# The fifth matmul of the first product on 64 array rows, two output tiles side by side

## What is computed

```python
w = exp(weight_gen - max);  w = w / (sum(w) + 1e-9)         # 8 heads, 7 taps
x = sum over 7 taps of w * (x shifted by the tap)            # 8192 x 192
h = maximum(x @ w_in1, 0);  x = (h * h) @ w_out1             # 192 -> 2048 -> 192
h = x @ w_in2;              out = (h * clip(h + 3, 0, 6) / 6) @ w_out2
```

## Time and profile before

| | |
|---|---|
| median of 3 runs | 1269.47 us |
| span of the profiled execution | 1266.2 us |
| TensorE matmul busy | 1228.9 us, 5536 matmuls |
| TensorE weight loads busy (beside the matmuls) | 1002.4 us |
| VectorE busy | 911.6 us |
| ScalarE busy | 655.9 us |
| GpSimd busy | 43.0 us |
| matmuls of the first product (line 601) | 2640 |

### The profile page before, as it was taken

One profiled execution on the slowest core, in us unless ns is written; L12 is line 12 of the kernel. 1 busy time (PEld: TensorE's weight loads), 2 busy tenths in 40 slices (PEclk: granted clock), 3 DMA queues, 4 the chain that ended last, 5 costly groups with the idle time before them and its releaser, 6 DMA issues.

```text
span 1266.2 us, 14912 instructions
## 1 busy us (share of the span) xinstructions
PE 1228.9 (97%) x5536; PEld 1002.4 (79%) x5536; DVE 911.6 (72%) x930; ACT 655.9 (52%) x732; POOL 43.0 (3%) x31
## 2 busy tenths in 40 slices
PE   2898999999999999999999999999999999999998
PEld 1886888888888888888888888888888888888886
DVE  8869777786777867677686777867677686776554
ACT  3774555545555554554555455454555545555554
POOL 4124000000000000000000000000000000000000
PEclk9899999999999999999999999999999999999999
DMA  5410000010000100000000000100000000000000
GB/s 154 128 44 17 32 17 32 0 45 2 16 31 0 47 0 16 31 16 31 0 27 20 16 31 0 47 0 16 31 16 31 0 16 31 12 0 1 13 1 25
DMA packets 12802, 31.43 MB, mean 25 GB/s; under 512 B 1140, under 2 KB 7666, under 8 KB 12784
## 3 DMA queue, kind: packets, MB, share of 16 engines
q1 hardware_dynamic: 12784, 31.19, 7.6%
HBM read 24.89 MB, written 6.29 MB: 25 GB/s over the span
## 4 chain that ended last, share of the span: by engine, by line
PE 92%; DVE 6%; issue 1%; ACT 1%; DMA 0%; SPq 0%; DVEq 0%; ACTq 0%
PE h_ps L601 45%; PE y_ps L622 9%; PE y_ps L627 9%; PE y_ps L624 9%; PE y_ps L623 9%; PE y_ps L626 9%; DVE acc L430 2%; DVE hid_lo L496 1%; DVE prod L443 1%; DVE hid L485 1%; PE y_ps L637 1%; PE y_ps L638 1%; PE y_ps L648 1%; PE y_ps L652 0%; DMA xwin<-in_x_dram 0%
## 5 line engine op out<-in xcount | busy, mean ns | idle before, releaser
L601 PE MATMUL h_ps<-xt,win 128*128 128x512 f32 (+1 forms) x2640 | 643.3, 390 | 1.4 <-DVE xt L478 1.4
L601 PEld LDWEIGHTS h_ps<-xt,win 128*128 128x128 f32 x2640 | 487.8, 190 | 109.2 <-DVE xt L478 1.8
L496 DVE TENSOR_TENSOR hid_lo<-hid,hid_hi 128x1024 fp32r<-128x1024 f32 (+1 forms) x262 | 314.6, 1201 | 167.5 <-ACT hid_hi L309 156.3
L309 ACT ACTIVATE hid_hi<-hid 128x1024 fp32r<-128x1024 f32 x246 | 261.0, 1061 | 287.1 <-DVE hid L487 155.6
L293 ACT ACTIVATE hid<-h_ps,three 128x1024 f32<-128x1024 f32 x128 | 143.2, 1119 | 141.7 <-PE h_ps L601 141.7
L485 DVE TENSOR_TENSOR hid<-hid 128x1024 f32<-128x1024 f32 x120 | 150.3, 1252 | 89.1 <-ACT hid L293 87.0
L487 DVE SCALAR_TENSOR_TENSOR hid<-hid,h_ps 128x1024 f32<-128x1024 f32 x128 | 156.0, 1219 | 80.6 <-ACT hid L293 78.3
L622 PE MATMUL y_ps<-hid_hi,wout 128*128 128x512 f32 (+1 forms) x524 | 204.5, 390 | 8.9 <-DVE hid_lo L496 8.7
L293 ACT ACTIVATE hid<-h_ps 128x1024 f32<-128x1024 f32 (+1 forms) x136 | 132.7, 976 | 149.0 <-PE h_ps L601 145.0
L624 PE MATMUL y_ps<-hid_lo,wout 128*128 128x512 f32 (+1 forms) x524 | 203.8, 389 | 0.0
L623 PE MATMUL y_ps<-hid_hi,wout 128*128 128x512 f32 (+1 forms) x524 | 203.6, 389 | 0.0
(11 more groups left out here) (58 smaller groups left out, 368.7 us busy)
## 6 DMA issues: line engine op xcount, KB each, us to landing
xwin<-in_x_dram SPq DMA_DIRECT2D x14, 960.0 KB
out_dram<-out_sb SPq DMA_DIRECT2D x15, 384.0 KB, 2.4
stage<-in_moe_w_out_dram SPq DMA_DIRECT2D x8, 384.0 KB, 3.4
stage<-in_moe_w_in_dram SPq DMA_DIRECT2D x4, 512.0 KB, 8.1
stage<-in_moe_w_in_dram SPq DMA_DIRECT2D x8, 256.0 KB, 5.1
wraw<-in_weight_gen_dram SPq DMA_DIRECT2D x16, 112.0 KB, 2.3
xwin<-in_x_dram SPq DMA_DIRECT2D x1, 768.0 KB
xwin<-in_x_dram SPq DMA_DIRECT2D x2, 283.5 KB
```

The costliest lines, as they stand in the source:

```text
L309: act.activation(hi, hid[:, slot, :, 0:width], ACT.Copy).then_inc(hi_done, 1)
L496: dve.tensor_tensor(lo, hid[:, slot, :, 0:width], hi.bitcast(fp32), ALU.subtract).then_inc(lo_done, 1)
L601: ins = pe.matmul(h_ps[:, s % 2, t, 0:width], w[:, wn, cols], src[:, xn, tokens], start=(n == 0), stop=(n == len(passes) - 1))
```

## The change

The fourth pass stays. The fifth leaves the list and becomes one matmul for each tile on half of the array's rows: tile 0 uses partitions 0 to 63 (weight plane 3, xt plane 2, which is hi there), tile 1 uses partitions 64 to 127 (weight plane 3, and a new xt plane 3, in which the hi part of values 128 to 191 lies on partitions 64 to 127). Both come at the end of the step, after the eight matmuls on 128 rows. The product of the two lo parts of the rest is no longer computed. ScalarE fills the new plane with one more copy per chunk and layer, and TensorE waits for it by two new semaphores, `x1_dup` and `x2_dup`.

```diff
-        xt = [sb(f"xt{n}", [P, 3, N], fp32r) for n in range(2)]
+        xt = [sb(f"xt{n}", [P, 4, N], fp32r) for n in range(2)]
...
             def split_x1_hi(c, dst, half=None):
                 act.activation(dst[0:REST, 2, cols], y1_ps[0:REST, 1, cols], ACT.Copy).then_inc(x1_hi, 1)
+                act.wait_ge(x1_hi, 2 * c + 4 if half is None else 2 * half + 2)
+                act.activation(dst[REST:P, 3, cols], dst[0:REST, 2, cols].bitcast(fp32), ACT.Copy).then_inc(x1_dup, 1)
...
             def split_x2_hi(c, dst):
                 act.activation(dst[0:REST, 2, :], y_rest[:, :], ACT.Copy).then_inc(x2_hi, 1)
+                act.activation(dst[REST:P, 3, :], y_rest[:, :], ACT.Copy).then_inc(x2_dup, 1)
...
             def hidden_sums(g, layer, s, src, gated_before, half=None):
-                passes = [(0, 0), (0, 1), (1, 0), (2, 2), (3, 2)]
-                for t in range(PAIR):
-                    cols = slice((PAIR * s + t) * P, (PAIR * s + t + 1) * P)
+                passes = [(0, 0), (0, 1), (1, 0), (2, 2)]
+                tiles = [slice((PAIR * s + t) * P, (PAIR * s + t + 1) * P) for t in range(PAIR)]
+                for t, cols in enumerate(tiles):
                     for n, (wn, xn) in enumerate(passes):
-                        ins = pe.matmul(h_ps[:, s % 2, t, 0:width], w[:, wn, cols], src[:, xn, tokens],
-                                        start=(n == 0), stop=(n == len(passes) - 1))
+                        pe.matmul(h_ps[:, s % 2, t, 0:width], w[:, wn, cols], src[:, xn, tokens],
+                                  start=(n == 0), stop=False)
+                for t, (cols, rows, xn) in enumerate(zip(tiles, (slice(0, REST), slice(REST, P)), (2, 3))):
+                    ins = pe.matmul(h_ps[:, s % 2, t, 0:width], w[rows, 3, cols], src[rows, xn, tokens],
+                                    start=False, stop=True, tile_position=(rows.start, 0))
                 ins.then_inc(mm1_done, 1)
...
                     if s == 0:
                         pe.wait_ge(x1_lo, 2 * i + 4)
+                        pe.wait_ge(x1_dup, i + 2)
                     if s == STEPS:
                         pe.wait_ge(x2_lo, 2 * i)
+                        pe.wait_ge(x2_dup, i)
```

## The result

The changed kernel takes 1307.61 us (median of 4 runs, 1307.02 to 1309.27) against 1269.35 for the kernel before: a ratio of 1.0317, interval 1.0297 to 1.0337. It is slower, as forecast, by 38 us where 74 were forecast; 1343 was too high, and 1307.6 lies inside the range of 1298 to 1382, nearest to rival 3 (1315). The profiled execution has a span of 1305.4 us, 39.2 more than before.

What follows compares the result with a forecast made beforehand. TensorE's matmul slots were taken as the bound. Full steps add 68.8 us and half steps 5.1, so +73.9 on the profiled 1266.2 gives 1340.1; with 3.3 from span to median, 1343 us, range 1298 to 1382.

Steps and rivals of the forecast that it cites:

- rival 3: At the 64-row matmuls, both weight loads run side by side: +0.1675 us a full step, 1315 us; chance 0.16.
- The bound: In the main loop, TensorE's time is the number of matmul slots times the spacing of their starts.
- s: TensorE's slot for a matmul of 512 columns, the spacing of starts in the main loop: 0.2325 us.
- Emptying and open loads (d, l) from the 64-row transposes: Passage between 128 and 64 rows, priced from line 652's transposes: 2d + 3l = 0.51 us a full step.
- d: Emptying of the array at each change between 128 and 64 rows: 0.09 us, twice a step.
- l: Load of an fp32r operand of 128 columns that nothing covers: 0.11 us, three times a step.
- A beside B in one slot: The 64-row matmuls A (rows 0 to 63, tile 0) and B (rows 64 to 127, tile 1) stream side by side.
- Rival 4: The second 64-row matmul follows the first, its load covered: +0.40 us a step, 1374 us; chance 0.16.
- B's load behind A's: The second 64-row matmul's weight load follows the first's, so that matmul starts 0.11 us later.
- The half steps: 16 steps with 256-column slots: +0.39 us each, three covered by a TensorE wait, 5.1 us in all.
- ScalarE's copies and the new waits at nothing: The extra copies (0.58 us each, 33 times) and semaphore waits lie beside TensorE's work: 0 us, at most 19.
- Rivals 1, 2 and 5: Packing pays: 1210 us, chance 0.09; loads made ahead of the emptying: 1258, 0.05; tile position without effect: 1269, 0.02.

Runs made afterwards that it cites:

- e3: The kernel before without the fifth matmul of tile 1, all on 128 rows: 1212.87 us, ratio 0.9567.
- e2: The changed kernel with each 64-row matmul right after its own tile's four full matmuls, two visits a step: 1463.64 us, ratio 1.1548.
- e7: The changed kernel with both 64-row matmuls ahead of the fourth matmuls, each loading only 64 of its 128 weight columns: 1295.78 us in one run.
- e1: The changed kernel with tile 1's 64-row matmul also on array rows 0 to 63, like tile 0's: 1361.19 us, ratio 1.0740.
- e4: The changed kernel with the ten 128-row matmuls of the kernel before; only the new plane, copies and waits are left: 1269.24 us, ratio 1.0017.
- e8: e6 with x's low half ahead of the hidden values' low half, and first-product waits right before its first matmul: 1220.08 us, ratio 0.9618.
- e6: The changed kernel with both products of the main loop and last eight steps wholly in pairs of 64-row matmuls: 1284.37 us, ratio 1.0144.

## Why the prediction was right, and where its sum was not

- **The bound.** TensorE's slots set the time. Right: e3 took out one of 20 and got 0.2325 us a step, the value of s.
- **Emptying and open loads (d, l) from the 64-row transposes.** Right in size: entry 0.33, exit 0.42 and 0.34 in the visit, 0.39 for a visit in e2, and the split into d and a load that goes with the columns in e7. That a gap at fp32 transposes of 64 columns also prices the passage of 512-column fp32r matmuls was the bold step, and it held. What the rows show is the gap of 0.09; that it is the array emptying is the reading of it.
- **A beside B in one slot.** Right: they start within 0.01 us; e1, which forbids it, costs one slot more. Rival 4 (one after the other) is out.
- **B's load behind A's.** This step failed. I took it from line 601's second load, 0.11 after the first, but those two go into the same rows. Into the same rows it is so here as well (e1: 0.29 for the two), into different rows both start at once. One l of 0.11 a step, 27 us in 248 steps, is most of what the forecast was too high. The forecast for a step was +0.2775; rival 3's was 2d + 2l - s = 0.1675; 0.159 was measured. I had the counter-argument (B's rows are free) and gave it 0.16; it should have had more, since the rule for the load has the same ground as the rule for the matmul, which I believed.
- **The half steps.** The other part: 5.1 us forecast, 3.6 by rival 3's sum, 1.1 measured. The price of a visit isn't what is off there: away from the waits, a half step went from 2.37 us (starts at 43.97 and 46.34) to 2.66 (42.21 and 44.87), so +0.29 where rival 3 has 0.28 and the forecast 0.39. The sum took three visits as covered and all else in the stage as unchanged, and that is what was off. TensorE's waits of the stage came to 4.8 us where they were 6.3, and the granted clock between 35 and 40 us was 0.81 where it was 0.52. The first wait for low halves begins 0.8 us later than before and ends 1.7 us earlier, so most of its 2.5 us is VectorE being done sooner, not visits in its cover. Why it is done sooner is open; in e4, which has no visit, that wait is 3.06 us.
- **ScalarE's copies and the new waits at nothing.** Nearly so: e4's ratio is 1.0017 (1.0005 to 1.0029), about 2 us.
- **Rivals 1, 2 and 5** (packing pays, loads ahead of the emptying, no effect) fell with the first look at the visit. The Trainium skill's distance of about 4 ns between the starts of packed matmuls ("TensorE: Matmul & The Clock Gate", Part 3) agrees with A and B here (0.01 us or less). It doesn't count the way in and out, which "TensorEngine Tiling (Array Packing)", Key Properties, names without a price. Here that price, 0.39 us a visit, was larger than the slot of 0.2325 us that it bought.

## What to carry to other kernels

Price a change of the array's row mode before packing: it is paid once per visit (here 0.39 us: emptied twice, and two weight loads that nothing covers), and packing gives back one slot for each pair (0.2325 us at 512 columns). By these numbers, an estimate, a visit has to hold at least two pairs, or the kernel has to stay in the mode; only the latter was run (e8). Here the price could be read from small matmuls on fewer rows that the kernel already had, by starts and by where their loads stand; the mean duration and the busy share don't show it. A step measured on one resource (loads into the same rows) says nothing on two (loads into different rows).

## What the runs showed that I had not expected

TensorE takes a matmul and a load on 64 rows every 0.116 us for a whole loop (38 matmuls and 38 loads in 4.41 us, e6; e8's pass fits the same rate) and runs both halves at the full rate of a slot, so a product on 128 rows can be split into two on 64 at no cost in slots. Here the two were always in different PSUM banks; no run had them in one. A load into rows at work is covered in 64-row mode too (e1), although the Trainium skill ("TensorE: Matmul & The Clock Gate", Part 3, What overlaps and what doesn't) lets a load overlap only where the row groups differ: the trace disagrees with that sentence. And a wait can cost more than its length: after ten of e6's 14 waits of about 3.2 us the clock fell for a while (0.68 in the mean over 4 us at the one shown), which made those passes 1.6 us longer than the others.
